# Eight accumulator banks for the mixing, and the token product moved ahead of the softmax sums, in a fused attention, MLP and soft-MoE kernel

## What is computed

```python
logits = x @ phi                       # 2304 x 32 slots, x is 2304 x 512
d = np.exp(logits - logits.max(0)); d /= d.sum(0) + 1e-9
slot_input = d.T @ x                   # 32 x 512: the product over all tokens
# eight experts, four slots each: relu(slot_input[e] @ w1[e]) @ w2[e]
c = np.exp(logits - logits.max(1)); c /= c.sum(1) + 1e-9
out = c @ slot_out                     # 2304 x 512: the mixing
```

## Time and profile before

| what | us |
|---|---|
| median of 3 runs | 823.66 |
| lowest and highest run | 822.15, 827.57 |
| profiled execution, its own time | 823.54 |
| its span in the profile | 821.7 |

### The profile page before, as it was taken

The page is one execution under the profiler, slowest core; times in us unless marked ns, Lnnn a source line. Parts: engine busy times, 40 slices in busy tenths (PEclk is TensorE's granted clock), DMA queues, the critical chain, the costliest instruction groups (busy, mean ns, idle before and its releaser), DMA issues.

```text
span 821.7 us, 16948 instructions
## 1 busy us (share of the span) xinstructions
PE 751.1 (91%) x5993; PEld 698.9 (85%) x5993; DVE 534.7 (65%) x1430; ACT 374.5 (46%) x903; POOL 376.8 (46%) x394
## 2 busy tenths in 40 slices
PE   3899978999999699999999989999998999996996
PEld 2788878998999689999999889999998999993552
DVE  5899966777677676777777577777675444434323
ACT  3677754545454554546364454545443222111113
POOL 2344335565655165656474164747460776620000
PEclk9999989999999999999999699999999999997995
DMA  4433313333333113333334013333320545497976
GB/s 97 99 85 103 98 33 86 90 90 84 89 98 107 39 53 82 88 95 88 88 88 117 17 45 88 88 89 93 96 65 26 167 148 194 136 346 277 402 307 230
DMA packets 96518, 96.77 MB, mean 118 GB/s; under 512 B 61296, under 2 KB 61296, under 8 KB 96432
## 3 DMA queue, kind: packets, MB, share of 16 engines
q1 hardware_dynamic: 96432, 95.66, 38.5%
HBM read 90.84 MB, written 4.79 MB: 116 GB/s over the span
## 4 chain that ended last, share of the span: by engine, by line
PE 64%; DVE 16%; issue 8%; ACT 4%; DMA 4%; POOL 2%; SPq 1%; DVEq 0%; ACTq 0%; POOLq 0%
PE mb L1041 43%; PE yb L944 4%; PE zb L963 4%; PE xb L990 4%; DVE prob L747 3%; DMA qk_in<-in_k 2%; DVE ptl L753 2%; DMA ring_b<-in_moe_w 2%; PE mb L1016 2%; DVE qs L711 2%; ACT prob L595 1%; DVE kl L715 1%; PE xb L924 1%; PE mb L1080 1%; PE zb L1136 1%
## 5 line engine op out<-in xcount | busy, mean ns | idle before, releaser
L1041 PE MATMUL mb<-xh,wih 128*128 128x288 f32 x512 | 163.5, 319 | 11.4 <-DVE hid L813 7.0
L1041 PE MATMUL mb<-gh,woh 128*128 128x288 f32 x512 | 157.5, 308 | 3.8 <-DVE hid L813 3.8
L1041 PE MATMUL mb<-xl,wih 128*128 128x288 f32 x512 | 155.3, 303 | 0.0
L1041 PE MATMUL mb<-xh,wil 128*128 128x288 f32 x512 | 155.0, 303 | 0.0
L1041 PE MATMUL mb<-gl,woh 128*128 128x288 f32 x512 | 151.0, 295 | 0.0
L1041 PE MATMUL mb<-gh,wol 128*128 128x288 f32 x512 | 151.0, 295 | 0.0
L554 POOL TENSOR_TENSOR gl<-hid,gh 128x288 fp32r<-128x288 f32 x128 | 113.1, 890 | 57.1 <-ACT gh L636 55.8
L571 POOL TENSOR_TENSOR wol<-stage,woh 128x512 fp32r<-128x512 f32 x64 | 82.5, 1288 | 120.0 <-DVE woh L705 120.0
L813 DVE SCALAR_TENSOR_TENSOR hid<-gate,mb 128x288 f32<-128x288 f32 x128 | 57.6, 452 | 103.4 <-ACT gate L642 101.8
L595 ACT ACTIVATE prob<-prob,m_row 64x576 f32<-64x576 f32 (+4 forms) x160 | 96.4, 604 | 59.4 <-DVE m_row L728 58.8
L571 POOL TENSOR_TENSOR wil<-stage,wih 128x512 fp32r<-128x512 f32 x64 | 82.6, 1291 | 81.9 <-DVE wih L705 81.9
(11 more groups left out here) (145 smaller groups left out, 1450.3 us busy)
## 6 DMA issues: line engine op xcount, KB each, us to landing
stage<-in_moe_w_in SPq DMA_DIRECT2D x64, 256.0 KB, 3.3
stage<-in_moe_w_out SPq DMA_DIRECT2D x64, 256.0 KB, 2.7
ring_a<-in_moe_w SPq DMA_DIRECT2D x16, 1024.0 KB, 7.5
ring_b<-in_moe_w SPq DMA_DIRECT2D x14, 1024.0 KB, 11.6
cum_b<-cum_dram SPq DMA_DIRECT2D x32, 288.0 KB, 4.1
qk_in<-in_q SPq DMA_DIRECT2D x32, 144.0 KB, 3.3
qk_in<-in_k SPq DMA_DIRECT2D x32, 144.0 KB, 3.7
v_in<-in_v SPq DMA_DIRECT2D x32, 128.0 KB, 3.3
```

The source lines that it names most:

```text
L1041: ins = mm(bank[:, 0:HALF], a[:, t, P * (j % 4):P * (j % 4) + P], x[:, t, cols], start=(i == 0), stop=(i == 11))
```

## The change

The mixing takes all eight PSUM banks in turn (`mix_ps`), and each of the 20 output tiles has a place of its own (`obuf[t]`, in `ring_a[0]` to `ring_a[2]`); a matmul waits for the copy of tile t - 8, no copy waits for a store, and all stores count on one semaphore. The product over all tokens waits for the exponential; the matmul for the sums is issued within it, behind tile 11. Tiles of 64 rows are multiplied with 64 rows. The clearing of `x2last` is gone, the `sel4` copies stand behind the subtraction, and the clearing of the two banks stands behind the sums' copies.

```diff
--- before.py
+++ after.py
@@ -272,7 +272,6 @@
         ox = sb("ox", [P, P], F32, tail_b)
         so4 = sb("so4", [P, MODEL], F32R, tail_b)
         tail_b.close()
-        NOUT = 8
 
         room = x2last[:, :, :].rearrange("p i n -> p (i n)")
         hx = room[:, 0:512].rearrange("p (e n) -> p e n", e=2)
@@ -281,7 +280,7 @@
 
         ring = ring_a + ring_b + [ring_x[:, :]]
         NR = len(ring)
-        obuf = ring_a[0][:, :].rearrange("p (i n) -> p i n", i=NOUT)
+        obuf = [ring_a[t // 8][:, MODEL * (t % 8):MODEL * (t % 8) + MODEL] for t in range(BATCH * QT)]
 
         cum_dram = nc.dram_tensor("cum_dram", (BATCH * HEADS, SEQ), F32).ap()
 
@@ -290,6 +289,7 @@
         yb = pb("yb")
         zb = pb("zb")
 
+        mix_ps = [bank[:, i, :] for bank in (mb, xb, yb, zb) for i in range(2)]
         xbf = xb[:, :, :].rearrange("p a n -> p (a n)")
         ybf = yb[:, :, :].rearrange("p a n -> p (a n)")
         qk_ps = xbf[:, QK_AT:QK_AT + SEQ]
@@ -304,7 +304,7 @@
         c_dma = [sem(f"c_dma{i}") for i in range(2)]
         w_dma = [sem(f"w_dma{i}") for i in range(2)]
         e_dma = [sem(f"e_dma{i}") for i in range(NR)]
-        out_dma = [sem(f"out_dma{i}") for i in range(NOUT)]
+        out_dma = sem("out_dma")
 
         const_made = sem("const_made")
         ident_zero = sem("ident_zero")
@@ -504,10 +504,8 @@
             for t in range(BATCH * QT):
                 b, i = t // QT, t % QT
                 sp.wait_ge(mixed_out[t % 2], t // 2 + 1)
-                sp.dma_start(out[SEQ * b + P * i:SEQ * b + P * i + QW[i], :], obuf[0:QW[i], t % NOUT, :]
-                             ).then_inc(out_dma[t % NOUT], 16)
-            for i in range(NOUT):
-                sp.wait_ge(out_dma[i], 16 * ((BATCH * QT - 1 - i) // NOUT + 1))
+                sp.dma_start(out[SEQ * b + P * i:SEQ * b + P * i + QW[i], :], obuf[t][0:QW[i], :]).then_inc(out_dma, 16)
+            sp.wait_ge(out_dma, 16 * BATCH * QT)
 
 
         @block.gpsimd
@@ -671,9 +669,7 @@
             nc.scalar.copy(so4[:, :], yb[:, 1, :]).then_inc(t_act, 1)
             for t in range(0, BATCH * QT, 2):
                 act.wait_ge(mixed, t + 1)
-                if t >= NOUT:
-                    act.wait_ge(out_dma[t % NOUT], 16 * (t // NOUT))
-                nc.scalar.copy(obuf[:, t % NOUT, :], zb[:, 0, :]).then_inc(mixed_out[0], 1)
+                nc.scalar.copy(obuf[t], mix_ps[t % 8]).then_inc(mixed_out[0], 1)
 
 
         @block.vector
@@ -830,11 +826,7 @@
             dve.wait_ge(l_kept, 2 * BATCH)
 
             nc.vector.tensor_reduce(gmax[:, :], gm[:, :, :].rearrange("p b s -> p s b"), AX_X, ALU.max).then_inc(t_dve, 1)
-            nc.vector.memset(x2last[64:P, 4, :], 0.0)
-
-            for i in range(4):
-                ins = nc.vector.tensor_copy(sel4[32 * i:32 * i + 32, :], ident[32 * i:32 * i + 32, 32 * i:32 * i + 32])
-            ins.then_inc(sel_made, 1)
+
             dve.wait_ge(t_pe, 1)
             nc.vector.tensor_reduce(smax[:, :], zb[0:SLOTS, 0, 0:P], AX_X, ALU.max).then_inc(t_dve, 1)
             dve.wait_ge(t_dve, 2)
@@ -843,14 +835,17 @@
             nc.vector.tensor_tensor(ew[:, :, :], logits[:, :, :],
                                     zb[:, 1, 0:SLOTS].unsqueeze(1).broadcast_to([P, BATCH * QT, SLOTS]),
                                     ALU.subtract).then_inc(t_dve, 1)
-            dve.wait_ge(token_out, 1 + BATCH * QT)
-
-            nc.vector.memset(mb[:, :, 0:256], 0.0)
-            nc.vector.memset(yb[:, 0, 0:P], 0.0)
+            for i in range(4):
+                ins = nc.vector.tensor_copy(sel4[32 * i:32 * i + 32, :], ident[32 * i:32 * i + 32, 32 * i:32 * i + 32])
+            ins.then_inc(sel_made, 1)
             dve.wait_ge(t_act, 1)
             nc.vector.tensor_reduce(es4[:, 0, :], ew[:, :, :].rearrange("p t s -> p s t"), AX_X, ALU.add).then_inc(t_dve, 1)
             dve.wait_ge(t_dve, 5)
             nc.vector.tensor_copy(es4[:, 1:4, :], es4[:, 0, :].unsqueeze(1).broadcast_to([P, 3, SLOTS])).then_inc(t_dve, 1)
+            dve.wait_ge(token_out, 1 + BATCH * QT)
+
+            nc.vector.memset(mb[:, :, 0:256], 0.0)
+            nc.vector.memset(yb[:, 0, 0:P], 0.0)
             dve.wait_ge(t_pe, 3)
             nc.vector.tensor_scalar(den[:, :], zb[:, 0, 0:1], EPS, None, ALU.add).then_inc(t_dve, 1)
             dve.wait_ge(t_dve, 7)
@@ -900,9 +895,7 @@
             nc.vector.tensor_tensor(so4[64:P, :], yb[64:P, 1, :], so4[64:P, :].bitcast(F32), ALU.subtract).then_inc(t_dve, 1)
             for t in range(1, BATCH * QT, 2):
                 dve.wait_ge(mixed, t + 1)
-                if t >= NOUT:
-                    dve.wait_ge(out_dma[t % NOUT], 16 * (t // NOUT))
-                nc.vector.tensor_copy(obuf[:, t % NOUT, :], zb[:, 1, :]).then_inc(mixed_out[1], 1)
+                nc.vector.tensor_copy(obuf[t], mix_ps[t % 8]).then_inc(mixed_out[1], 1)
 
 
         @block.tensor
@@ -1050,15 +1043,18 @@
             tr(zb[0:SLOTS, 0, 0:P], gmax[:, :], ident[:, :]).then_inc(t_pe, 1)
             pe.wait_ge(t_dve, 3)
             mm(zb[:, 1, 0:SLOTS], ones[0:SLOTS, :], dmax[:, :], start=True, stop=True).then_inc(t_pe, 1)
-            pe.wait_ge(t_dve, 6)
-            mm(zb[:, 0, 0:1], es4[:, :, :].rearrange("p r s -> p (r s)"), ones[:, 0:1], start=True, stop=True).then_inc(t_pe, 1)
+            pe.wait_ge(t_act, 1)
             pe.wait_ge(token_out, 1 + BATCH * QT)
 
             nt = BATCH * QT
             for t in range(nt):
-                x = x2tok[:, t, :] if t < 3 * QT else x2last[:, t - 3 * QT, :]
-                g = t % 4
-                ins = mm(xb[32 * g:32 * g + 32, 0, :], ew[:, t, :], x, start=(t < 4), stop=(t >= nt - 4))
+                r, g = QW[t % QT], t % 4
+                x = x2tok[0:r, t, :] if t < 3 * QT else x2last[0:r, t - 3 * QT, :]
+                ins = mm(xb[32 * g:32 * g + 32, 0, :], ew[0:r, t, :], x, start=(t < 4), stop=(t >= nt - 4))
+                if t == 11:
+                    pe.wait_ge(t_dve, 6)
+                    mm(zb[:, 0, 0:1], es4[:, :, :].rearrange("p r s -> p (r s)"), ones[:, 0:1], start=True, stop=True
+                       ).then_inc(t_pe, 1)
             ins.then_inc(t_pe, 1)
 
             pe.wait_ge(t_dve, 9)
@@ -1131,9 +1127,9 @@
             pe.wait_ge(t_dve, 11)
             pe.wait_ge(c_trc, BATCH)
             for t in range(nt):
-                if t >= 2:
-                    pe.wait_ge(mixed_out[t % 2], t // 2)
-                mm(zb[:, t % 2, :], ct4[:, t, :], so4[:, :], start=True, stop=True).then_inc(mixed, 1)
+                if t >= 8:
+                    pe.wait_ge(mixed_out[t % 2], (t - 8) // 2 + 1)
+                mm(mix_ps[t % 8], ct4[:, t, :], so4[:, :], start=True, stop=True).then_inc(mixed, 1)
 
 
 _INS = ["q", "k", "v", "f", "moe_w_in", "moe_w_out", "moe2_phi", "moe2_w1", "moe2_w2"]
```

## The result

The changed kernel took 832.36 us (median of 11 runs, 829.35 to 836.85), the kernel before 826.28 us beside it (median of 11 runs, 817.83 to 828.97). The ratio is 1.0128 with a 95% interval of 1.0095 to 1.0160: slower by 1.3%, or 10.6 us (7.9 to 13.2). A ratio uses only runs within about 1.5% of the fastest of their kernel, so it can lie up to 0.6% off the ratio of the medians, which here is 1.0074 (6.1 us). That the change is slower doesn't hang on this: each of its 11 runs took longer than each of the 11 of the kernel before. The prediction said 822.4 us and no difference that could be measured. The profiled execution took 830.16 us (span 828.1).

The account below looks back on a forecast made before the run. The prediction took weight DMA to bound the expert stage after the product, and nothing alone to bound the mixing. From 823.54 us, + 1.8 (later product end) - 2.9 (mixing) gave 822.4 us, its own range 820.0 to 824.3.

Parts of the forecast that it names:

- Start of the product: Product over all tokens: it waits for the exponential alone and starts at 747.9 instead of 751.0, 3.1 us earlier.
- Slots and changes: 64-row tiles in the product break its ten slots into 16 to 18; shape changes cost 0.1 to 0.15 us each.
- I keep 4.3 us at the low clock: Product over all tokens: 4.3 us of it run at 1.2 GHz, as before, the rest at 2.4 GHz.
- Rival (b): Product over all tokens: the clock doesn't come back, product 18.4 us, 8.6 later, 829.2 us in all; chance 0.08.
- the expert stage moves one for one with the end of the product: Expert stage, bound by DMA: it shifts exactly as the product's end does, forecast 1.8 us late.
- Mixing: Last stage: eight banks let TensorE run on until DMA bounds the stage; 2.9 us gained.
- Rival (c): Mixing: the eight banks bring nothing, since queued writes hinder one another; 825.3 us in all; chance 0.07.
- Rival (a): Product over all tokens: the 64 rows cost nothing, it keeps ten slots; 818.2 us in all; chance 0.33.

Follow-up runs that it names:

- the filled kernel: Changed kernel plus 24 small matmuls that compute nothing that is read, placed in TensorE's waits ahead of the product: 833.00 us, ratio 1.0191.
- the first kernel of the last table: Changed kernel with 128 rows, last batch's softmax ahead of VectorE's wait for the sums, 24 unused matmuls before the product and 10 behind: 819.04 us, ratio 1.0019.

## Why the prediction was wrong

- **Start of the product: right.** 3.0 us against a forecast of 3.1. The `sel4` copies (L839) ended before the exponential, as forecast, and the sums' matmul made nobody wait.
- **Slots and changes: right.** One of the forecast's two cases was 18 slots in nine pairs; the timeline has them in that order. A lone slot is 0.855 us at 1.2 GHz (0.86). Where a change of shape follows, the two slots take 1.84 to 1.87 us instead of 1.71 (eight times), so a change costs 0.13 to 0.16 us, against a forecast of 0.1 to 0.15.
- **The step that failed: "I keep 4.3 us at the low clock".** It was all 17.25 us. 18 x 0.855 is 15.4, with the changes 1.2 and 0.5 for L1056 it makes 17.1. The forecast's product had 11.6 us (747.9 to 759.5), so the clock made 5.6 us of the miss; the kernel in which broken sets did get the clock back, with one-column matmuls, roughly bears the 11.6 out (11.8 us without the added pairs, 6.6 of them at the low clock). Rival (b) had the mechanism right, with 18.4 us for the product and 829.2 us in all. That its total fell within 1 us of the profiled execution, 830.16, is partly luck: its product was 1.1 us too long, it had nothing for the slower experts (2.9 us, next point), and the untouched part ran 1.2 us shorter. I gave it 0.08, on the ground that TensorE would still work more than three quarters of the time. It worked all of the time, and that brought no clock. The trace of before could not tell this; but it held no 64-row pass among column groups, and I priced an unseen form by busy share. That should have taken the chance of (b) up to that of the forecast, since the earlier trace rows had shown the clock coming back inside the product and nowhere else.
- **The second: "the expert stage moves one for one with the end of the product".** It lost 2.9 us more. L1063 took 1.91 us instead of 1.08 and the first `up` product 3.54 instead of 1.91, 2.5 us together, both at the low clock (the other 0.4 us I can't name). With the product late, the buffers had been full for long: the DMA engines slowed to 226 GB/s and then stood idle (0 in the third row of the stretch table), TensorE waited for no weights behind it, and so its own speed counted. The earlier trace rows showed TensorE idle 0.80 us for weights; here that DMA bound turned into a TensorE bound with the late start.
- **Mixing: right.** 2.9 us forecast, 2.9 measured in the profile. Rival (c) is out: the kernel with nothing but the mixing changed has the stage at 17.23 us.
- **Rival (a)**, 5.3 us faster than before with whole sets, wasn't this kernel. It is the kernel with 128 rows: 0.64% or 5.3 us faster, ends of the interval 2.6 and 8.1 (4.6 us by medians), and tail 4.9 us shorter. Its price was right, its premise ("The 64 rows cost nothing") holds only if no 128-row tile stands between them.

Shown: the 64-row tiles between the others cost the whole loss (one edit takes it away, one edit alone brings it), and rearranged they cost nothing that the timed runs show. Supported by three profiles with 64-row passes between the others and three without (changed groups, one-column matmuls, lone passes of 128 rows), but not settled: that the 64-row passes are what keeps the clock down, rather than lone passes of any form. Not tried: a 64-row product at the full clock throughout, and the old mixing at the full clock.

## What to carry to other kernels

A matmul with fewer rows isn't a cheaper matmul: a lone pass of 512 columns took 0.85 us at 1.2 GHz with 64 rows and with 128, and among 128-row tiles that share the array side by side a 64-row tile breaks the set. Keep forms together, the odd ones in a set of their own, or pay with full rows. When an edit breaks up a dense stretch of TensorE within which the clock used to come back, price the stretch and what follows it at the low clock first, and only then ask whether it will recover.

## What was not expected of the hardware

- TensorE busy 9.29 of 9.30 us and 7.46 of 7.50 us without the clock leaving 1.2 GHz, and in the filled kernel a fall of the clock with 1.80 of 1.80 us busy. The Trainium skill, TensorE: Matmul & The Clock Gate, Why this matters for your kernels, advises keeping TensorE continuously busy for the highest throughput. By that the clock should have come back within this product. The trace disagrees.
- A change between 128 and 64 rows costs 0.13 to 0.16 us at 1.2 GHz, by the length of the pairs above.
- Four 64-row passes in the four column groups stream side by side as 128-row ones do.
- The timed executions of one kernel spread by 7.5 to 24 us, and the clock was lost and regained at other places in each profile: regained at 755.3 before and at 748.3 with 128 rows, and in the first kernel of the last table not lost in the tail until behind the mixing's last matmul. Differences under 3 us can't be read from a dozen runs here.
